# Attention and a two-stage mixture of experts on one core: routing per batch inside attention, and experts over blocks of 512 tokens

## What is computed

```python
for t in range(S):                                  # attention, S = 768
    S_re, S_im = ar * S_re - ai * S_im + k[t] v[t], ar * S_im + ai * S_re
    y[t] = q[t] @ S_re
logits = x @ w_gate + modality_bias[modality_id]    # 3072 x 8
e = argmax(logits); p = softmax(logits)[e]
x = p * (relu(x @ w1[e]) @ w2[e])                   # 384 -> 1024 -> 384
out = ((x @ m1) * (x @ m2)) @ w3 @ w_out            # 384 -> 1024 -> 1024 -> 384
```

## Time and profile before

| | |
|---|---|
| median of three executions | 1190.52 us (1188.71 to 1190.99) |
| profiled execution | 1191.97 us, of it the span 1190.1 us |
| granted TensorE clock, mean | 0.965 |
| PE busy | 906.0 us, 76% |
| DVE busy | 434.5 us, 37% |
| ACT busy | 299.5 us, 25% |
| POOL busy | 159.9 us, 13% |
| read and written in DRAM | 49.29 and 14.18 MB |

### The profile page before, as it was taken

How to read it: one execution, slowest core, us unless ns; L and a number is a source line. 1 busy time by engine, 2 the same in 40 slices (tenths; PEclk the granted TensorE clock), 3 DMA queues, 4 the chain that set the end, 5 groups by cost and what they waited for, 6 DMA issues and landing times.

```text
span 1190.1 us, 13549 instructions
## 1 busy us (share of the span) xinstructions
PE 906.0 (76%) x4642; PEld 650.1 (55%) x4643; DVE 434.5 (37%) x759; ACT 299.5 (25%) x496; POOL 159.9 (13%) x186
## 2 busy tenths in 40 slices
PE   0000002998999937758899999999979999999997
PEld 0000001677778823434455555555558898988986
DVE  2699998586773310533011111111141111120110
ACT  6800012344443314102210110110142222231221
POOL 0000000000000012262000000000033232332322
PEclk9999999998999969889899999999999999999999
DMA  9020005376646233567400000000000000000000
GB/s 373 0 80 0 0 0 121 119 201 161 177 126 176 65 92 106 221 237 218 157 1 0 0 0 0 0 0 0 0 1 7 20 20 7 26 0 27 14 14 27
DMA packets 43683, 83.09 MB, mean 70 GB/s; under 512 B 8672, under 2 KB 30328, under 8 KB 41592
## 3 DMA queue, kind: packets, MB, share of 16 engines
q1 hardware_dynamic: 33480, 67.08, 18.5%
q0 software_dynamic: 3072, 9.46, 2.1%
q10 hardware_dynamic: 7088, 5.97, 2.0%
HBM read 49.29 MB, written 14.18 MB: 53 GB/s over the span
## 4 chain that ended last, share of the span: by engine, by line
PE 54%; DMA 3%; issue 2%; another core or an unknown queue 2%; ACTq 1%; ACT 1%; DVE 0%; SPq 0%; POOL 0%; POOLq 0%; DVEq 0%
PE moe_bank L1432 11%; PE moe_bank L1449 11%; PE moe_bank L1471 8%; PE moe_bank L1473 8%; PE moe_bank L1472 8%; PE moe_bank L1441 2%; DMA x<-w_out 2%; PE moe_bank L1402 1%; DMA mid_w<-x_sorted 1%; PE moe_bank L1372 1%; ACTq L1037 1%; PE moe_bank L1479 1%; PE moe_bank L1364 1%; PE moe_bank L1412 0%
## 5 line engine op out<-in xcount | busy, mean ns | idle before, releaser
L525 PE MATMUL bank<-consts 128*128 128x512 f32 x40 | 19.6, 643 | 199.8 <-DVE gates L461 199.8
L1432 PE MATMUL moe_bank<-expert_w,shared 128*128 x312 | 140.1, 599 | 3.1 <-POOL shared L969 3.1
L1449 PE MATMUL moe_bank<-expert_w,shared 128*128 x416 | 138.5, 486 | 1.9 <-DVE shared L1294 1.9
L525 PEld LDWEIGHTS bank<-consts 128*128 128x128 f32 x40 | 8.0, 208 | 208.6 <-issue 208.6
L1338 DVE TENSOR_TENSOR u_sb<-a_sb,moe_bank 128x512 f32<-128x512 f32 x48 | 33.0, 687 | 235.1 <-PE moe_bank L1473 235.1
L1471 PE MATMUL moe_bank<-x2T_hi,mid_hi 128*128 128x512 f32 x288 | 112.9, 392 | 3.5 <-DVE x2T_lo L1321 3.5
L1449 PEld LDWEIGHTS moe_bank<-expert_w,shared 128*128 128x128 f32 x416 | 79.0, 190 | 62.3 <-issue 14.1
L1473 PE MATMUL moe_bank<-x2T_hi,mid_lo 128*128 128x512 f32 x288 | 112.9, 392 | 0.0
L1472 PE MATMUL moe_bank<-x2T_lo,mid_hi 128*128 128x512 f32 x288 | 112.7, 391 | 0.0
L1304 DVE TENSOR_TENSOR x<-x,moe_bank 128x384 f32 x26 | 14.4, 554 | 243.7 <-PE moe_bank L1449 243.7
L1059 ACT ACTIVATE shared<-moe_bank,step_gate 128x512 f32<-128x512 f32 x52 | 35.7, 687 | 250.0 <-PE moe_bank L1432 250.0
(11 more groups left out here) (169 smaller groups left out, 1434.1 us busy)
## 6 DMA issues: line engine op xcount, KB each, us to landing
ks<-mags SPq DMA_DIRECT2D x48, 144.0 KB, 3.0
expert_w<-w SPq DMA_DIRECT2D x4, 1536.0 KB
qs<-gates SPq DMA_DIRECT2D x42, 146.2 KB, 4.3
gates<-a_re SPq DMA_DIRECT2D x4, 1170.0 KB, 12.3
gates<-a_im SPq DMA_DIRECT2D x4, 1170.0 KB, 14.6
mid_w<-x_sorted ACTq DMA_DIRECT2D x24, 193.0 KB, 2.5
v_in<-v SPq DMA_DIRECT2D x8, 576.0 KB, 5.0
spare<-k SPq DMA_DIRECT2D x4, 1152.0 KB, 5.2
```

What stands on the lines that cost most here:

```text
L525: nc.tensor.matmul(bank[:, :], cst("ident"), const[:, 0:512], start=True, stop=True)
L1432: mm = nc.tensor.matmul(bank[h][:, :], xt[s][:, k], expert_w[:, bass.ds(slot + (k * F + h * HF), HF)], start=(k == 0), stop=(k == KD - 1))
L1449: mm = nc.tensor.matmul(bank[4 + s][:, 0:DM], hidT[s][:, k], expert_w[:, bass.ds(slot + (W1C + k * DM), DM)], start=(k == 0), stop=(k == K ...
```

## The change

Token order, routing and the expert loop are written anew; the mathematics of attention and of the closing layer stays.

- **Routing inside attention.** `turn_y` multiplies by a matrix that holds the identity and the gate's weights (`gate_pairs`), so that rows and their part of the logits come out of the same two matmuls. ACT keeps both (two copies). x stays in SBUF (`rows(b)`); the store to DRAM and the reload go. DVE chooses the experts of a batch (`choose`, `gate`, `place`), PE ranks its tokens in each expert (`route_ranks`: 7 or 8 small matmuls), POOL scatters its six tiles (`route_scatter`), each expert into a region of its own of 3072 rows in `x_sorted`. Batches 0 to 2 are done beside the units of later batches, batch 3 after the last unit. Then DVE builds a table of 13 steps (`tables`).
- **The zeroing matmul** (L570 before) goes: the first state matmul starts the bank.
- **The fold** of w3 and w_out moves ahead of attention, beside the prefix products; the folded weights are split there and stored to DRAM (`lw_hi`, `lw_lo`) by POOL, which also zeroes 512 rows of each region.
- **The flag** is found inside the last batch; its column is turned to a row by a transfer through DRAM.
- **Experts in blocks of 512 tokens.** A step of the table is one block of one expert. The x rows are loaded from the region, scaled by their gate, turned, split. The weights of every block are loaded anew, split in two passes (ACT the high, DVE the rest), and are the stationary side; all matmuls are split ones of 512 columns. The output comes out transposed and is kept in `x2T`, from which the closing layer takes its operand without transposes. SP copies the ids of each block to `order` in DRAM, and loads them back once.
- **The closing layer** has its six blocks written out, its weights split beside the last expert block, and the folded weights loaded back.

The core of the diff, attention first:

```diff
             def turn_y(g):
...
                 for q in range(HU // 2):
-                    mm = nc.tensor.transpose(bank_y[:, q, 0:PAIR], yT[:, q], ident_pair)
+                    mm = nc.tensor.matmul(bank_y[:, q], yT[:, q], L.gate_w[0:PAIR, m, q], start=True, stop=True)
...
-                            else:
-                                nc.tensor.matmul(bank_s[0:SD, 0:HU * WIDE], const[SD:SD + 1, 0:SD], const[SD:SD + 1, 0:HU * WIDE],
-                                                 start=True, stop=True)
+                            elif n in RANKS_AT:
+                                pe.wait_ge(R.rank_read, RANKS_AT[n] + 1)
...
             turn_y(B * NU * NCH - 1)
+            route_ranks(nc, pe, L, R, B - 1, rank)
...
+            pe.wait_ge(w3_in, 2 * DMA)
+            for f in range(KF + 1):
+                if f < KF:
...
+                    for k in range(KF):
+                        mm = nc.tensor.matmul(psum[f % 2][:, 0:DM], L.w3T[:, k, f * P:(f + 1) * P], L.w_out[:, k],
+                                              start=(k == 0), stop=True, skip_group_check=True)
...
+            for f in range(KF):
+                pool.wait_ge(lw_ready, 2 * f + 2)
+                pool.dma_start(io["lw_hi"][:, f], L.early_hi[:, f % 2].bitcast(F32)).then_inc(lw_stored[f % 2], DMA)
+                pool.dma_start(io["lw_lo"][:, f], L.early_lo[:, f % 2].bitcast(F32)).then_inc(lw_stored[f % 2], DMA)
...
             load_k(0)
             load_q(0)
+            for i in range(2):
+                sp.wait_ge(lw_stored[i], KF * DMA)
+            sp.wait_ge(zero_stored, E * DMA)
...
+            V.choose(B - 1)
+            V.gate(B - 1)
+            V.read_rank(B - 1)
+            V.place(B - 1)
+            V.tables()
```

Its helper on PE, and the loops of PE, ACT and DVE in the experts:

```diff
+def route_ranks(nc, pe, L, R, r, rank):
...
+    nc.tensor.matmul(rank[:, 0:NB * E], L.rcst("before"), L.hot[:, r].rearrange("p c e -> p (c e)"), start=True, stop=True,
+                     skip_group_check=True)
+    for i in range(NB - 1):
+        nc.tensor.matmul(rank[:, (i + 1) * E:NB * E], ones, L.hot[:, r, i:i + 1].broadcast_to([P, NB - 1 - i, E]),
+                         start=False, stop=True, skip_group_check=True)
...
+            def hidden(j):
+                pe.wait_ge(xT_lo_ready, j * KD + KD)
+                for f in range(KF):
+                    cols = slice(f * P, (f + 1) * P)
+                    if f >= 2:
+                        pe.wait_ge(hid_lo_ready, j * KF + (f - 1))
+                    pe.wait_ge(w1_lo_ready, j * KF + (f + 1))
+                    for k in range(KD):
+                        mm = split_matmul(bank_hid[f % 2][:, :], w1_hi[:, k, cols], w1_lo[:, k, cols], xT_hi[:, k], xT_lo[:, k],
+                                          k == 0, k == KD - 1)
+                    mm.then_inc(hid_psum, 1)
...
+            with pe.Fori(0, NS - 2) as i:
+                with pe.If(runs(pe, i + 2)):
+                    output(i + 1, 0, i * KD + 1)
+                    turn_x(i + 2)
+                    output(i + 1, 1, i * KD + 2)
+                    output(i + 1, 2, i * KD + 3)
+                    hidden(i + 2)
...
+            def hidden_highs(j):
+                for f in range(KF):
+                    act.wait_ge(hid_psum, j * KF + (f + 1))
+                    nc.scalar.activation(hid_hi[:, f], bank_hid[f % 2][:, :], ACT.Relu).then_inc(hid_hi_ready, 1)
+                    if f == 0:
+                        act.wait_ge(w2_in, j * DMA + DMA)
+                    nc.scalar.copy(w2_hi[:, f], stage2[:, f]).then_inc(w2_hi_ready, 1)
...
+                    scale_x(i + 1)
+                    w1_highs(i + 1, w1_in, w1_hi_ready)
+                    x_highs(i + 1)
+                    hidden_highs(i + 1)
...
+            def keep(j, at, d):
+                dve.wait_ge(out_psum, j * KD + (d + 1))
+                nc.vector.tensor_copy(x2T[:, d, bass.ds(at, BLOCK)], bank_out[d][:, :]).then_inc(x2T_kept, 1)
...
+                    w1_lows(i + 1, w1_hi_ready, w1_lo_ready)
+                    keep(i, at, 0)
+                    x_lows(i + 1)
+                    keep(i, at, 1)
+                    keep(i, at, 2)
+                    hidden_lows(i + 1)
```

1403 lines of the change are left out of this document (731 added, 672 removed).

## The result

| | before | after |
|---|---|---|
| median | 1190.76 us (1188.71 to 1190.99, 4 runs) | 1032.48 us (1030.28 to 1033.65, 4 runs) |
| ratio | | 0.8672, 95% interval 0.8653 to 0.8691 |
| forecast | | 1005 us, range 990 to 1042 |
| profiled execution, span | 1191.97, 1190.1 | 1033.65, 1031.8 |
| granted TensorE clock, mean | 0.965 | 0.928 |

Faster, as forecast, and within the range, but 27 us above the forecast: 158 us were gained where 185 were expected. The forecast's sum for the span was 1004.6 us; the span measured is 1031.8.

A forecast was written before the change was run, and what follows sets the result against it. The prediction saw a chain of stages feeding PE unequally. Start through attention 422.3, attention's extra 6, tail 32, experts 240.4, closing layer 296.2 and end 7.7 summed to a 1004.6 us span, 1005 us as median; range 990 to 1042.

The forecast's parts named there:

- the turn of y: Attention: turning y back takes two more instructions 48 times; up to 10 us, 4 taken, since DVE fills the units.
- 17 steps of a 512-column matmul on split words take 3.85 us, 0.2265 us each: Step price from PE's timeline before the change, used for the experts' blocks: 144 matmuls, 32.6 us each.
- Six iterations of the loop run empty ... so 2 us is taken, 0 to 5 possible: Experts, after the last block: empty loop turns priced at 2 us within the stage's 240.4 us.
- no gap before the closing layer: Sign that the forecast is right: PE goes from the experts to the closing layer without a gap.
- Leaving the stage and testing the flag took 5.2 us: Tail between attention and experts: took the tail from +18 to about +21 us, within 32 us for 153.1.
- Sum +6 us: Attention: net of zeroing matmul removed, turning y back, rank groups and their reading; ends -5 and +20 us.
- The fold under the prefix: Before attention: folding weights while PE and ACT are free, ending near 150 us, costs nothing.
- The rival of late stores: Before attention: POOL's stores wait for the prefix's end, +50 us, 1055 us; chance 0.08 shared with late ids.
- Bank waits: Rival, experts' hidden layer: PE waits for its banks, 0.4 us 56 times, +22 us, 1027 us; chance 0.13.
- the low clock: Rival, experts: waits keep PE at 1.2 GHz, +201 us, 1206 us; chance 0.02 shared with empty blocks being run.
- cheaper case: Attention at -5 us and the tail at 26 us give 994 us; chance 0.10.
- the first (attention and its tail dearer, 1032 us): Rival: attention and the tail after it at their dear ends, +14 and +13 us, 1032 us; chance 0.17.

The follow-up runs named there:

- e2: The changed kernel with the w1 tiles and the hidden words moved to start 352 bytes above a multiple of 512: 1021.92 us.
- e4: The changed kernel with all engines' block loops ending at seven, so no empty turns: 1022.76 us.
- e6: The changed kernel without the never-entered fallback function recurrence and the reading of its flag: 1028.53 us.
- e11: The changed kernel with the matmul that turns y back issued three times a chunk in place of two: 1044.59 us.
- e8: The changed kernel with the first six or seven rank matmuls of each of three groups inside attention run twice: 1038.97 us.
- e12: The changed kernel with ACT's and DVE's eight splitting passes over w1 made twice from the second block on: 1032.57 us.
- e7: The changed kernel with one whole-word f32 matmul in place of three split ones in the experts: 1087.75 us in one execution.
- e9: The changed kernel with w1 and hidden words moved to 352 and loops in two parts, blocks eight to thirteen behind one test: 1016.69 us.

## Why the prediction came out as it did

The mechanisms were right in the main. The sum was 27.2 us short: one price did not hold in the new layout, and three covers were not there, that of the empty turns, that of leaving attention and that of the turn of y.

- **"17 steps of a 512-column matmul on split words take 3.85 us, 0.2265 us each".** This price was carried to all split matmuls of the new layout, and failed there: 0.2335 where w1 or w2 are the weights, because of where the tiles lie. e2 gives it back, 10.6 us by the medians: all of the closing layer's 4.8, and 0.9 us in each block of the experts, about 6 of their 13.7.
- **"Six iterations of the loop run empty ... so 2 us is taken, 0 to 5 possible".** They cost 7.5 us, outside the bounds, and with the slow steps behind the idle stretch 9.3 (e4: 9.7 by the medians). The cover was wrong. Before, the gap that priced it was this one (timeline of PE):

```profile
866.62 5.42 PE L1449 MATMUL moe_bank<-expert_w,shared 128*128 x16 [1.93 <-DVE shared L1294]
```

and the three empty turns ahead of it were these (PE's stream, from 860.8 to 866.5 us):

```profile
L866 PEldq TENSOR_LOAD <-table x3: 300/302/310, 861.0 to 863.8; - x3
```

A turn took 1.4 us there too, but the three ran while PE had matmuls left until 864.7 us. Here six took 8.2 us, and PE had work for 2.2 of them. This is the other half of the experts, and it breaks one of the prediction's own signs, "no gap before the closing layer": the gap stands ahead of the last output.

- **"Leaving the stage and testing the flag took 5.2 us".** The price was near, 5.7 us here, but its start was wrong: the prediction had the scatters landed at +18 us and the experts begun at about +21, so that most of the leaving ran beside the landing. It began only when POOL had drained, at +18.6 (e6), and the first instruction of the experts came at +24.2. From there to the first transfer of x (458.09 to 459.79) lie 1.7 us more that had no term. These two are the 5 us of the tail. The rest of the working held: positions at +7.0 us (440.87, forecast +6.5), the table at +15.2 (+15).
- **Attention, "Sum +6 us".** It grew by 11.5. The term that was mis-sized is the turn of y: two more instructions a chunk, for which the prediction took 4 us and allowed 10. A further two cost 12.1 us by the medians, and 5.3 in the five units at clock 1.00 alone (e11). The reason given for 4, that DVE fills the units, fails: the turn stands on PE's path in each of them. The other two terms came out near their price by the medians: the rank groups 6.5 (7), though e8 doubles only most of their matmuls and not their reading, and the zeroing matmul -6.6 (-5). That the three add up to 12.0 is in part luck, since the clock of the third and fifth unit is in every one of these medians. In units 1, 2, 6, 7 and 8, at clock 1.00 in all five columns of the table, attention grew by 7.5 us, and the terms measured there give 5.5: 5.3 for the turn, 2.9 for the ranks, -2.7 for the zeroing. What the other 2 us are, no run shows; the second copy per chunk on ACT, priced at nothing, and the reading of the ranks were not tested.
- **The end**, 5.8 us for 7.7, was not studied.

What held:

- *The fold under the prefix* was priced at nothing and cost nothing; it ended at 116 us, not 150, since a group of 16 took 5.4 to 6.3 us and not the 10.3 of the low clock. The rival of late stores (1055 us) is out. The rule of the Trainium skill (SBUF — State Buffer, "SBUF: two separate sides" and "Who interferes with whom") that exempts tensor_tensor agrees: transfers from POOL's queue landed in 2.2 and 2.4 us (medians) beside a DVE full of tensor_tensor.
- *Bank waits* (1027 us) did not appear: 1.4 us of idle time ahead of all hidden matmuls, and e12 shows room beside them.
- *The ids* were in time: the page gives 7.7 us from issue to landing, and PE has no gap in the closing layer.
- *The blocks*: seven of them, the granted clock 0.98 over the whole stretch, so neither the low clock (1206) nor empty blocks (1208). The prediction's reading that matmuls step slowly "just after an idle spell" was loose: in the timeline of before five quicker steps stand between the idle stretch (to 877.88 us) and the first slow one (879.15).
- *The split and the transposed output*: e7 puts 53.5 us in the experts down to the split of the words, more than the 48.4 that the stage gained; the blocks of 512 alone gained next to nothing there.

The prediction's cheaper case was added up wrongly: attention at -5 for +6 and the tail at 26 for 32 are 17 us less, 988 us and not 994, below the range.

Of the rivals, the first (attention and its tail dearer, 1032 us) happened by 10.5 of its 27 us. That the time lies where it and the rival of the banks (1027) put it is luck in the larger part: two prices that no rival named, the step and the empty turns, make about 18 us of the difference (10.6, and 9.3 less the 2 that were taken). Reading the median alone would have confirmed the wrong cause.

## What to carry to other kernels

A price taken from a matmul's row holds for the layout it was measured in: where operands move, measure the step again, and give tiles that meet on PE the same start modulo 512 bytes, which here cost nothing and was worth 10.6 us of 1032 (9.7 of them on PE's path from the experts on). A loop over the largest possible count, with a test inside, is not free where PE has nothing left to do: here six empty turns cost 9.7 us (e4), and they stand where the next stage waits. When a stage is cut to a few tens of us, list every jump between functions that it contains and what the engines wait for ahead of it: here a skipped function took 5.7 us, and that began only when POOL's last scatters had drained.

## What the runs showed of the hardware that was not expected

- A matmul of 512 columns of split words steps by 0.227 or by 0.234 us at the same granted clock, by the distance between the starts of its two operands in SBUF: 0 and 256 modulo 512 bytes are short, 32, 96, 128 (there at 384 columns), 384 and 448 long, and 64 lies between (0.229).
- An empty turn of a loop (a word of the table read, a branch over the body) took PE's stream 1.4 us, before and in the change; the branch over the body took 0.2 us of it in the change. One branch over a longer skipped stretch of code took far more: 3.75 us in e9, 4.1 over the recurrence in the change, 3.8 over that of before.
- POOL's drain behind a row of scatters ended 4.0 us after the last of them, in the change and in e6, and held all engines that long.
- After 7.5 us of idle time PE made nine steps at 0.43 us, the 1.2 GHz level (granted clock 0.52), before the step fell back to 0.23; fourteen after 7.6 us in e2, and seven after 3.8 us in e9.
